# A 128-point transform that multiplies the high part with both tables at once, one tile a slot later

## The reference

```python
X = np.fft.fft(x, axis=1)
X = np.fft.fft(X, axis=2)
u = x + np.real(X)
un = (u - mean(u)) / np.sqrt(var(u) + 1e-06)
return u + np.maximum(un @ w_ch1, 0.0) @ w_ch2
```

## Time and profile before

| | |
|---|---|
| median of 3 runs | 1250.38 us |
| the profiled execution, own time | 1252.61 us |
| its span | 1250.8 us |
| TensorE matmul busy | 1220.3 us (98%) |
| TensorE weight loads busy | 1195.4 us (96%) |
| VectorE busy | 821.7 us (66%) |
| ScalarE busy | 645.5 us (52%) |
| GpSimd busy | 425.4 us (34%) |
| mean granted TensorE clock | 0.992 |

### The profile page before, as it was taken

One profiled execution on the slowest core, in us unless ns is written; L12 is line 12 of the kernel. 1 busy time (PEld: TensorE's weight loads), 2 busy tenths in 40 slices (PEclk: granted clock), 3 DMA queues, 4 the chain that ended last, 5 costly groups with the idle time before them and its releaser, 6 DMA issues.

```text
span 1250.8 us, 23662 instructions
## 1 busy us (share of the span) xinstructions
PE 1220.3 (98%) x8448; PEld 1195.4 (96%) x8448; DVE 821.7 (66%) x2191; ACT 645.5 (52%) x1603; POOL 425.4 (34%) x542
## 2 busy tenths in 40 slices
PE   6799999999999999999999999999999999999998
PEld 5799999999999999999999999999999999999998
DVE  5565576777775577655557777765666777766654
ACT  5355555444465555445555555544445555554553
POOL 0133342343343254333333244421212344533331
PEclk9899999999999999999999999999999999999999
DMA  9857543344556532224434322222323233222220
GB/s 290 279 197 228 180 143 91 104 132 138 162 182 214 181 123 90 74 69 134 135 97 138 115 92 87 92 68 81 96 88 106 84 103 92 92 93 86 86 68 29
DMA packets 87677, 154.46 MB, mean 123 GB/s; under 512 B 11448, under 2 KB 46627, under 8 KB 87516
## 3 DMA queue, kind: packets, MB, share of 16 engines
q1 hardware_dynamic: 79944, 133.95, 33.8%
q0 software_dynamic: 7616, 18.99, 4.7%
HBM read 94.59 MB, written 63.32 MB: 126 GB/s over the span
## 4 chain that ended last, share of the span: by engine, by line
PE 92%; DMA 2%; DVE 2%; issue 1%; POOL 1%; SPq 1%; ACT 1%; POOLq 0%; ACTq 0%
PE bank L800 20%; PE bank L801 9%; PE bank L781 8%; PE bank L788 7%; PE bank L789 7%; PE bank L785 7%; PE bank L782 7%; PE bank L837 4%; PE bank L804 4%; PE bank L890 3%; PE bank L853 2%; PE bank L913 2%; PE bank L855 2%; PE bank L854 2%; PE bank L874 2%; PE bank L803 2%
## 5 line engine op out<-in xcount | busy, mean ns | idle before, releaser
L985 ACT ACTIVATE ht<-bank 128x384 fp32r<-128x384 f32 x528 | 258.9, 490 | 509.4 <-PE bank L789 504.1
L1169 DVE SCALAR_TENSOR_TENSOR ht<-bank,ht 128x384 fp32r<-128x384 f32 x528 | 293.7, 556 | 342.7 <-ACT ht L985 333.5
L800 PE MATMUL bank<-w,ht 128*128 128x384 f32 x1320 | 418.7, 366 | 0.8 <-DVE ub L1177 0.5
L801 PE MATMUL bank<-w,ht 128*128 128x192 f32 x1320 | 331.1, 251 | 0.0
L1417 POOL TENSOR_TENSOR ub<-ub,tmp 128x576 f32<-128x576 f32 x88 | 125.8, 1429 | 461.1 <-DVE ub L1177 310.9
L800 PEld LDWEIGHTS bank<-w,ht 128*128 128x128 f32 x1320 | 248.9, 189 | 4.0 <-issue 3.1
L801 PEld LDWEIGHTS bank<-w,ht 128*128 128x128 f32 x1320 | 252.5, 191 | 0.0
L781 PE MATMUL bank<-uth,w1h 128*128 128x384 f32 x528 | 189.4, 359 | 0.0
L785 PE MATMUL bank<-utl,w1h 128*128 128x384 f32 x528 | 179.2, 339 | 0.3 <-DVE utl L1194 0.2
L788 PE MATMUL bank<-uts,w1s 128*128 128x384 f32 x528 | 178.9, 339 | 0.3
L782 PE MATMUL bank<-uth,w1l 128*128 128x384 f32 x528 | 178.8, 339 | 0.0
(11 more groups left out here) (118 smaller groups left out, 2219.6 us busy)
## 6 DMA issues: line engine op xcount, KB each, us to landing
f1t<-f_copy SPq DMA_DIRECT2D x44, 396.0 KB
ub<-x_two SPq DMA_DIRECT2D x44, 288.0 KB
mix<-mixed SPq DMA_DIRECT2D x44, 288.0 KB, 3.2
out<-ub SPq DMA_DIRECT2D x44, 288.0 KB
xin<-in_x SPq DMA_DIRECT2D x12, 864.0 KB, 7.2
x_conv<-xin SPq DMA_DIRECT2D x12, 756.0 KB
vch<-v_split SPq DMA_DIRECT2D x42, 192.0 KB
mixed<-rowk SPq DMA_DIRECT2D x88, 74.2 KB
```

The lines of the kernel that those rows point to most:

```text
L800: e.matmul(dn[t][:, 0:2 * D], hh, w2[ph][:, m, :], start=(m == 0), stop=False)
L801: mm = e.matmul(dn[t][:, 0:D], hl, w2[ph][:, m, 0:D], start=False, stop=False)
L985: e.activation(hth[q % 4], up[q % 3][:, 0:TOK], ACT.Relu).then_inc(act_h, 1)
L1169: e.scalar_tensor_tensor(htl[q % 4], up[q % 3][:, 0:TOK], 0.0, hth[q % 4].bitcast(F32), ALU.max, ALU.subtract).then_inc(dve_l, 1)
```

## The change

- **One load, both tables.** `dft_tile` does one tile: x2h's 128 channels are loaded once and multiplied with a moving operand of 2 x 132 columns (both table parts side by side), x2l's 128 channels are loaded and multiplied with the table's high part, added to the first 132 columns; the other 64 channels keep three matmuls of 132 columns. So 5 matmuls for a tile in place of 6, and a tile fills one bank: columns 0 to 263 on 128 partitions, columns 264 to 395 on 64.
- **Emptying.** ScalarE copies per tile (2 instructions, 6 for a unit). VectorE subtracts per tile (2 instructions) and, as the product of x2h and the table's low part now stands apart, adds it in a third one, after a wait on its own `dve_zl`: 9 instructions for a unit. All of them move 132 elements per partition, each 33 elements from the last.
- **Slots.** Tiles 0 and 1 (banks 0 and 1) stay where the unit stood; tile 2 (bank 0) follows right after `up_slot` of the next slot. The last two units of a batch, and the convolution pieces of batch 2, stand in other slots, and `part_of_t` takes bank 1.
- **Put-off units.** Six instead of seven; the folded tile is stored (one DMA of 288 KB rather than two), fetched five slots or so ahead into `xf`, and split then.

```diff
-PUT_OFF = 7
+PUT_OFF = 6
...
+                if w in later:
+                    put_at[slot_after(*fold_at[w], 2)] = w
+                    spot = (n1 + 1 + u // 2, u % 2 * 3)
+                    made, third = slot_after(*spot, -1 if u % 2 == 0 else -2), slot_after(*spot, 1)
+                elif u < NB - 2:
+                    made, spot, third = [(n0 + u + 2, m) for m in (2, 4, 5)]
+                elif u == NB - 2:
+                    made, spot, third = (n1 - 1, 5), (n1, 0 if b else 1), (n1, 1 if b else 3)
                 else:
-                    dft_at[spot] = w
+                    made, spot, third = [(n1, m) for m in ((1, 3, 4) if b else (3, 4, 5))]
...
             for m in range(M6):
+                if (n, m) in third_at:
+                    fill(("dft", third_at[(n, m)], 2), 0, True)
...
                 if (n, m) in t_part:
-                    fill(("t",) + t_part[(n, m)], 0, False)
+                    fill(("t",) + t_part[(n, m)], 1, False)
...
+            def dft_tile(w, t):
+                k = dft_order.index(w)
+                if t == 0:
+                    e.wait_ge(f1_in[k % 2], (k // 2 + 1) * 16)
+                    e.wait_ge(dve_x2l, k + 1)
+                bk, q = empty(e, ("dft", w, t))
+                xh, xl, wave, both = x2h[:, t], x2l[:, t], f1t[:, k % 2, 0, t, :], f1t[:, k % 2, :, t, :]
+                e.matmul(bk[:, 0:4 * KC].rearrange("p (a c) -> p a c", a=2), xh[:, 0:128], both, start=True, stop=False,
+                         skip_group_check=True)
+                e.matmul(bk[:, 0:2 * KC], xl[:, 0:128], wave, start=False, stop=True, skip_group_check=True)
+                o = bk[0:64, 4 * KC:6 * KC]
+                e.matmul(o, xh[:, 128:D], wave, start=True, stop=False, skip_group_check=True)
+                e.matmul(o, xh[:, 128:D], both[:, 1], start=False, stop=False, skip_group_check=True)
+                e.matmul(o, xl[:, 128:D], wave, start=False, stop=True, skip_group_check=True).then_inc(pe_tb[q], 1)
...
+            def spectrum_high(w, t):
+                if w == 0 and t == 0:
                     e.wait_ge(v_stored[1], 16)
+                o, q = full(e, ("dft", w, t))
+                copy(spectrum_rows(zh[:], w, t), spectrum_part(o, 0))
+                copy(spectrum_rows(zs[0:64], w, t), spectrum_part(o[0:64], 2)).then_inc(act_tb[q], 1)
...
+            def spectrum_low(w, t):
+                o, q = copied(e, ("dft", w, t))
+                low, rest = spectrum_rows(zl[:], w, t), spectrum_rows(zs[64:128], w, t)
+                e.tensor_tensor(low, spectrum_part(o, 0), spectrum_rows(zh[:], w, t).bitcast(F32), ALU.subtract)\
+                    .then_inc(dve_zl, 1)
+                e.tensor_tensor(rest, spectrum_part(o[0:64], 2), spectrum_rows(zs[0:64], w, t).bitcast(F32), ALU.subtract)
+                e.wait_ge(dve_zl, dft_order.index(w) * TB + t + 1)
+                e.tensor_tensor(low, spectrum_part(o, 1), low.bitcast(F32), ALU.add).then_inc(tb_free[q], 1)
...
+            def put_off(w):
+                e.wait_ge(dve_xf, w + 1)
+                e.dma_start(x2s[later.index(w)], xf[:, w % NB % 2]).then_inc(x2_out[w % NB % 2], 16)
+
+            def fetch(w):
+                e.wait_ge(x2_out[w % NB % 2], (later.index(w) // 2 + 1) * 16)
+                xf_free(e, w, "fetched")
+                e.dma_start(xf[:, w % NB % 2], x2s[later.index(w)]).then_inc(x2_in[w % NB % 2], 16)
```

More of the change, by code:

```diff
@@ L324, in program @@
+                made_at[made], dft_at[spot], third_at[third] = w, w, w
         dft_order = [dft_at[spot] for spot in sorted(dft_at)]
[L327 to L330, removed]
+        assert dft_order == [third_at[spot] for spot in sorted(third_at)] == [made_at[spot] for spot in sorted(made_at)]
@@ new lines, in program @@
+        made_of = {w: spot for spot, w in made_at.items()}
+        xf_before = {}
+        for half in range(2):
+            held = [(spot, w, "folded") for w, spot in fold_at.items() if w % NB % 2 == half]
+            for w in later[half::2]:
+                ahead_ = max((made_of[v], v) for v in fold_at if v % NB % 2 == half and made_of[v] < made_of[w])
+                fetch_at[slot_after(*ahead_[0], 1)] = w
+                held.append((slot_after(*ahead_[0], 1), w, "fetched"))
+            held.sort()
+            for k in range(1, len(held)):
+                xf_before[held[k][1:]] = held[k - 1][1:]
@@ L998, in x2_high @@
             def x2_high(w):
-                e.wait_ge(dve_xf, w + 1)
-                x2_free(e, w, "made")
+                if w in later:
+                    e.wait_ge(x2_in[w % NB % 2], (later.index(w) // 2 + 1) * 16)
+                else:
+                    e.wait_ge(dve_xf, w + 1)
+                x2_free(e, w)
                 copy(x2h[:], xf[:, w % NB % 2]).then_inc(act_x2h, 1)
@@ L1197, in turned_low @@
                     .then_inc(tb_free[q], 1)
-            def xf_free(w):
-                before = max([v for v in range(w) if v % NB % 2 == w % NB % 2], default=-1)
-                wait(e, act_x2h, before + 1)
-                wait(e, dve_x2l, before + 1)
             def fold_sum(n):
```

121 lines of the change are left out of this document (52 added, 69 removed).

## The result

The changed kernel takes 1285.05 us (median of 4 runs, 1283.02 to 1287.89) against 1250.36: 1.0284 times as long, 95% interval [1.027, 1.0298], 34.7 us more. Forecast were 1274 (23.7 more) and 1245 to 1285. The direction and the mechanism were right, the size was not, and the range missed the time by 0.05 us.

A forecast was written before the change was run, and what follows sets the result against it. The prediction took TensorE to bound the kernel. Its terms, 9.2 + 5.5 - 0.8 + 6.2 + 1.3 + 2.3, summed to +23.7 us: 1276.3 for the profiled execution, 2.2 above the median, so 1274; range 1245 to 1285.

The forecast's parts named there:

- Tile of 0.36, 264 columns 0.12: TensorE's new tile: the 264-column matmul takes 0.12 us, four more 0.06 each, 0.36 in all.
- Saved 0.33 per unit: TensorE's matmuls: 0.33 us less per unit, 14.5 us over 44 units if nothing else waited.
- Triple of 1.28, no overlap: VectorE's zl, zs, zl per tile don't overlap: 1.28 us from start to bank free.
- Regular unit +0.57: Units with low_rank behind tile 2: waits of 0.19 and 0.71 against 0.33 saved; 16 units, +9.2 us.
- part_of_t +0.68: Units with part_of_t in slot 5, which waits 0.82 for bank 1: 0.68 us each, 8 units, +5.5 us.
- Nothing behind: -0.14: Six units with neither low_rank nor part_of_t behind them: 0.19 wait less 0.33 saved each, -0.8 us.
- Batch ends +2.05: Last units of batches 1 to 3: waits on VectorE's x2_low, turn and banks, 2.05 us per batch, +6.2 us.
- Put-off units +2.3: Six put-off units, blocks 23 to 25: waits 8.4, less 2.0 saved, less 4.1 from early fetch, +2.3 us.
- Table load one slot later, nothing: Table load still two slots or more before its use: no cost; if late, 44 times a few tenths.
- Storing folded, nothing; x2h and x2l out of blocks 13 to 18, nothing: One store DMA for two, off the chain; x2_high and x2_low moved where TensorE isn't waiting: no effect.
- Rival 2: Banks come free in time, if bank 0's chain is 0.7 shorter: TensorE's saving stays, 1232 us; chance 0.15.
- Rival 3: TensorE's clock falls too after new waits at batch ends and put-off blocks: 1283 us and above; chance 0.13.

The follow-up runs named there:

- e7b: The changed kernel with SyncE issuing the table load first in its slot, ahead of the store and the load that waits for GpSimd; 1285.99 us.
- e2: The changed kernel with the five emptying instructions of a tile moving 8 elements per partition instead of 132 in batches 1 to 3; 1257.69 us.
- e3: The changed kernel with VectorE's second instruction per tile writing to partitions 0 to 63 instead of 64 to 127 in batches 1 to 3; 1270.96 us.
- e4: The changed kernel with the transform and emptying of the kernel before (18 matmuls in one slot), all other edits kept; 1255.55 us.
- e5b: As e4, but with the convolution pieces of batch 2 in the slots of the kernel before; 1254.17 us.
- e8b: As e5b, with SyncE issuing the table load first in its slot; 1254.52 us.
- e12b: The kernel before with the 5-matmul tile in 27 units only, tile 0 in slot 3, tiles 1 and 2 in slot 4; 1262.64 us.
- e9b: The changed kernel with the convolution pieces of batch 2 in the slots of the kernel before; 1283.63 us.
- e6b: The changed kernel with the emptying instructions writing 132 neighbouring elements per partition, not every 33rd, in batches 1 to 3; 1263.89 us.

## Why the prediction was right or wrong

- *Tile of 0.36, 264 columns 0.12.* Right within 0.02 (0.38 and 0.13). The chain in block 44 of e7b's kernel, whose tiles are those of the changed one, unit 10's tile 2 with nothing to wait for:

```profile
734.13 0.13 PE bank L867
734.26 0.06 PE bank L869
734.32 0.06 PE bank L871
734.39 0.07 PE bank L872
734.46 0.06 PE bank L873
```

- *Saved 0.33 per unit.* Right: 0.32 in e2's blocks 57 to 64. The estimate from the Trainium skill ("TensorE: Matmul & The Clock Gate", section Back-to-back issue gap), 0.05 saved per tile and so 0.15 per unit, is not what these blocks show; the measurement decides.
- *Triple of 1.28, no overlap.* Right: 0.43 + 0.41 + 0.40 = 1.24; e3 shows that the partition of the output is the reason, and that it is worth 14 us. This is the rule of the Trainium skill ("VectorE: DVE Perf Modes", section Two Vector instructions with no wait between them), by which an output that starts in another quadrant of 32 partitions than the last one is held; the trace agrees (0.43 and 0.41 between starts, 0.31 and 0.30 in e3).
- *Regular unit +0.57.* Measured +0.46 to +0.56 in blocks 58 to 64; low_rank cost 0.67 to 0.70 (forecast 0.71), and slot 5 grew by 0.55 where e2, in which nothing waits, has 0.41: 0.14 of wait for tile 2 (forecast 0.19). *part_of_t +0.68*: 0.59 (slot 4 -0.73, slot 5 +1.32).
- *Nothing behind: -0.14.* Partly wrong. The unit itself gives -0.17, but unit 7 of batches 2 and 3 is followed by 0.9 in slot 0 of the next block, a wait that had no term: TensorE's down matmul waits for VectorE's add_residual, now behind tile 2. Timeline of the changed kernel at the start of block 65:

```profile
999.78 0.40 DVE L1252 TENSOR_TENSOR zl<-bank,zl 128x132 fp32r<-128x132 f32 x1
...
1000.08 0.88 DVE L1201 TENSOR_TENSOR ub<-bank,ub 128x192 f32<-128x192 f32 x3
...
1000.58 0.42 PE L820 MATMUL bank<-w,ht 128*128 128x384 f32 x1 [0.72 <-DVE ub L1201]
```

  In the regular blocks the same wait is hidden, as low_rank's comes first.
- *Batch ends +2.05.* Right within 0.4: blocks 44 and 66 grew by 2.25 and 2.20, where the sum has 0.87 + 1.9 - 0.25 - 2 x 0.33 = 1.86 for units 9 and 10. Unit 10's first tile waits 1.03, not 0.75. About half of it is the price of the new slot by itself: e4, e5b and e8b show 1.1 per end with before's transform. With unit 7's 0.9 the ends (columns 43-44 and 65-66) come to 3.0 where 1.9 was forecast: 2.2 us of the miss.
- *Put-off units +2.3*: this is the step that failed. It was "8.4 - 2.0 - 4.1 = +2.3", the 4.1 being the stall at 399.85 us, the clock behind it and smaller waits, which the early fetch was to give back. It gave back nothing net: with before's transform and the new fetch (e5b), blocks 22 to 25 are +0.4, +0.2, -1.7 and +1.4. The wait for the fetch went, and as much came back where the put-off units now stand: at the very place of the stall e5b still waits 1.03 in place of 1.37, now for x2l, which VectorE makes only one slot ahead and ends at 401.32, 0.10 before the matmul; in block 25 the same wait is 0.96 (its slot 0: +0.9). The chain of waits of e5b, and its timeline of VectorE:

```profile
400.39 1.03 issue
401.42 0.30 PE bank L870
...
400.56 0.76 DVE L1239 TENSOR_TENSOR x2l<-xf,x2h 128x576 fp32r<-128x576 f32 x1
```

  And part of the 4.1 never was a steady cost. In e12b, which has before's code there, the stall stands at 405.67 us (1.62), and TensorE's granted clock behind it stays at 1.00, where it was 0.50 (1.2 of 2.4 GHz) in the earlier trace rows; block 24 is 1.3 shorter with nothing changed in it. The sum also took 2.2 off at its end, by which the profiled execution was above the median; if the clock fall is part of those 2.2, it was credited twice. Windows of e12b, 3 us from 1 us after the stall (columns as in the earlier trace rows):

```profile
408.30:411.30 3.00, 3.00 (x26) 2.84 (x26) 1.17 (x2) 1.59 (x3) 1.61 (x6) 1.00 0.93 293
```

  The waits (8.4 gross there) were about right: e9b less e5b is 10.2 in blocks 19 to 27, where 0.57 + 2.05 + 8.4 - 2.0 = 9.0 was forecast. With 0.57, 2.05 and the pieces' 2.4 taken off, the put-off units cost 8.3 where 2.3 was forecast.
- *The convolution pieces of batch 2 and part_of_t in other slots* had no term. They cost 2.1 to 2.4 in blocks 19 to 27, and part of it goes back in blocks 11 and 12.
- *Table load one slot later, nothing.* Right, by e7b. *Storing folded, nothing; x2h and x2l out of blocks 13 to 18, nothing.* Right: no block from 13 to 18 differs by more than 0.15 in any version.

The 8.4 us missed in blocks 19 to 27 (13.3 for 4.9) are thus: the credit 4.1 + 0.7 (what e5b shows there in place of it), the pieces 2.4, the waits 1.2. The three add up by construction, as they are differences between the same kernels. That the late x2l ate what the fetch gave back is read from the rows above; no run made x2l earlier. Blocks 20 to 25, before and then changed: length, then the busy time of TensorE, its loads, VectorE, ScalarE and GpSimd.

```profile
330.86:436.20 105.34, 103.05 (x726) 99.30 (x725) 64.04 (x154) 63.46 (x149) 39.42 (x53) 0.98 0.63 201
```

```profile
341.26:456.36 115.10, 101.72 (x678) 92.75 (x677) 87.03 (x227) 71.78 (x192) 39.64 (x53) 1.00 0.47 151
```

VectorE goes from 61% to 76% of the stretch. It is busier still at the batch ends (91% of blocks 43 and 44). Rival 2 (faster) didn't come, as the chain is not 0.7 shorter; where it was made shorter the rival's mechanism is there (blocks 57 to 64: -1.3 in e6b, -2.6 in e2), but with dense writes in three batches of four the whole is still slower. Rival 3's clock fall did not come: the granted clock is 1.00 there, and 0.994 over the span.

Left open: e5b's median is 4.9 above before's, while its touched columns sum to 2.6 (before's profiled execution had 1.3 in block 24 that e12b's lacks; the other 1 us isn't placed).

## What to carry to other kernels

A matmul saved can be worth nothing if the bank it fills takes longer to empty than TensorE stays away from it: price the whole chain from the last matmul to the next use (copy, every VectorE instruction at its start-to-start distance, what is queued ahead of it), and do it for each user of the bank. When edits are moved into other slots, price each against VectorE's queue of that slot, even those that "only" change places. Do not count a stall seen once, or a clock fall behind it, as a gain; ask first what will stand there instead, and whether another execution shows it too.

## What the runs showed of the hardware

- VectorE's overlap of neighbours depends on the output's partition: 0.31 between starts with all outputs from partition 0, 0.43 and 0.41 with the middle one from partition 64, for the same durations of 0.40 (e3).
- 132 elements written 33 apart cost VectorE 0.40 and ScalarE 0.47 (on 64 partitions), against 0.29 and 0.27 dense (e6b).
- A VectorE subtraction with both inputs in SBUF, 0.75 us in e12b's rows above, took 1.94 us while GpSimd ran one of 768 elements; tile 0's emptying stood behind it, and block 8 became 2.4 (changed) to 3.9 (e7b) longer, where blocks 4 and 6 became 1.3 longer. The kernel before has the same pair (1.92 us at 171.16). Timeline of the changed kernel:

```profile
176.31 2.40 POOL L1497 TENSOR_TENSOR w1t<-w1t_raw,w1s 128x768 fp32r<-128x768 f32 x1
...
177.38 1.94 DVE L1239 TENSOR_TENSOR xf<-ub 128x576 f32<-128x576 f32 x1
```

That the two share a path is argued from their overlap in time and not tested.
